# A fused attention, channel-mix and gated-convolution kernel: the second pair of chunks reordered, and half of a first-layer product placed inside the attention

## The chip, the cores and the metric

The kernel runs on 1 core of one Trainium2 chip (8 cores). The metric is the device time of one execution in microseconds (us); before the change it is 277.2 us, the median of 3 runs (276.21 to 277.38).

## The reference

Three layers follow one another on 2 sequences of 768 tokens, 512 features, in fp32.

```
# 1. linear attention with a decay per head; 8 heads of 64, blocks
intra = (q k^T * lam^(i-j), i>=j) v
inter = (q * lam^(i+1)) state
state = lam^block * state + (k * lam^(block-1-j))^T v
x     = intra + inter                      # (B, S, 512)
# 2. channel mix
xk = mu_k*x + (1-mu_k)*x_prev ; xr = mu_r*x + (1-mu_r)*x_prev
x2 = sigmoid(xr @ w_r) * (relu(xk @ w_k)**2 @ w_v)       # w_k: 512 x 1024
# 3. gated convolution
out = (sigmoid(conv5(x2)) * (x2 @ w_val)) @ w_out
```

## The kernel before

**Tiling.** The attention works on 12 chunks of 128 tokens (chunks 0 to 5 are the first sequence, 6 to 11 the second), two chunks being a pair p = 0 to 5. Everything behind it works on 3 tiles t of 512 tokens, so tile 0 needs pairs 0 and 1 alone. Each large product is done in three passes (`three_pass`, L714): every fp32 operand is split into a rounded high part and a low part (raw minus high), and high*high, low*high and high*low are added up in one PSUM bank. ScalarE (ACT) writes the high parts, VectorE (DVE) the low ones.

**Chunk n on TensorE (PE):** `scores(n)` (L725, 8 matmuls of k against q, two heads at a time), `update(n)` (L745, the new part of the state), `inter(n)` (L770, state times decayed q; none for chunks 0 and 6), `attend(n)` (L789, v times weighted scores). Chunks 5 and 11 have no update. Update n writes bank 6 (n even) or 7 (n odd). A pair's result lies in banks 4 and 5 (pair 5: 0 and 1) and is copied out by ACT (`evacuate_x`, L322).

**Chunk n on the other engines.** DVE: `weigh(n)` (L502, two 128x512 products that turn scores into pT) and `new_state(n)` (L512, faded state plus update). ACT: `fade(n)` (L333, four small activations that fade state n by the decay of a chunk). So the state goes update, new_state, fade, new_state, from chunk to chunk. GpSimd (POOL): `decay_k` and `decay_q` (L280, L291), which make kdec and qd from loaded k and q.

**Tile 0 of the channel mix** is prepared within the attention: `mix_part` (ACT, L346), `mix` (DVE, L527), `mix_high` (ACT, L358), `mix_low` (DVE, L535) make xk and its two parts for k = 0 to 3, and `high` (ACT, L341) and `low` (DVE, L540) split the weight piece by piece. Piece i of w_k serves output groups 2i and 2i+1 of `hidden(t, n)` (L810, 12 matmuls of 128x128 by 128x512; n = 0 to 7). `hidden(0, 0)` already stands between the halves of pair 5.

**What sets the order.** Each engine runs one stream written out by hand; engines meet at counting semaphores alone (`wait_ge`), and a waiting instruction holds all behind it on its engine. All loads are issued by SyncE on one queue in the order of the code (L229 to L262). DVE's stream in the attention is the loop at L630, ACT's is L418 to L447, PE's is L888 to L925. Behind the attention, PE runs hidden, `receptance` (L831) and `value` (L840) of the three tiles and then the last layer.

Of the kernel before, what the change touches and what calls it, by code (L numbers as in the profile page):

```python
# [9 lines left out]
ALU = mybir.AluOpType  # L10
# [25 lines left out]
TURNED = 7  # L36
OUT_FIRST = 4


# [13 lines left out]
def build(nc, prm_in, qk_in, v0_in, kv_in, w_k, w_v, w_r, w_val, w_out, out):  # L53
    with ExitStack() as ctx:
# [146 lines left out]
        def bank_of(kind, t, n):  # L201
            if kind == "mlp":
                return (2 * FT * t + n + 2) % 8
            place_of = [("val", 0), ("val", 1), ("proj", 0), ("val", 2), ("proj", 1), ("proj", 2)].index((kind, t))
            return (4 * place_of + n + 2) % 8
# [4 lines left out]
        def _(sp):  # L210
# [31 lines left out]
            for p in range(3, NP - 1):  # L242
                load_qk(2 * p)
                load_qk(2 * p + 1)
                load_kv(2 * p)
                load_kv(2 * p + 1)
            load_qk(NCH - 2)
            load_qk(NCH - 1)
            load_weight(wk_raw, w_k, 0, wk_here)
            load_kv(NCH - 2)  # L250
# [70 lines left out]
        def _(act):  # L321
            def evacuate_x(p):  # L322

                b, c = at(2 * p)
                cols = slice(b * SEG + HALO + c * CH, b * SEG + HALO + (c + 2) * CH)
                first = out_banks(2 * p)[0]
                act.wait_ge(att_done, 2 * p + 2)
                if p == OUT_FIRST:
                    act.wait_ge(inter_done, inters(2 * p + 1))
                nc.scalar.copy(x[:, :, cols].rearrange("p (g a) i -> p g a i", g=2),  # L330
                               ps[:, first:first + 2, :].rearrange("p g (a i) -> p g a i", a=2)).then_inc(x_ready, 1)
# [91 lines left out]
            fade(3)  # L423
            evacuate_x(1)
            fade(4)
            for k in range(KT):
                mix_part(0, k, 0)
            evacuate_x(2)
            fade(7)
            for k in range(3):  # L430
                mix_high(0, k, 0)
            fade(8)
            evacuate_x(3)
            high(wk, wk_raw, 0, wk_here, wk_hi)
            fade(9)
            mix_high(0, 3, 0)
            high(wk, wk_raw, 1, wk_here, wk_hi)
# [63 lines left out]
        def _(dve):  # L501
# [33 lines left out]
            def mix_low(t, k, which):  # L535
                to, raw, hi, lo = ((xk, xk_f, xk_hi, xk_lo), (xr, xr_f, xr_hi, xr_lo))[which]
                dve.wait_ge(hi, KT * t + k + 1)
                nc.vector.tensor_tensor(to[1][:, k, :], raw[:, k, :], f32(to[0][:, k, :]), ALU.subtract).then_inc(lo, 1)

            def low(w, raw, i, hi, lo):  # L540
                cols = slice(i * PIECE, (i + 1) * PIECE)
                dve.wait_ge(hi, i + 1)
                nc.vector.tensor_tensor(w[1][:, cols], raw[:, cols], f32(w[0][:, cols]), ALU.subtract).then_inc(lo, 1)
# [84 lines left out]
            dve.wait_ge(halo_ok, B)  # L628
            dve.wait_ge(om_ok, 1)
            for p in range(2, NP):  # L630
                new_state(2 * p)
                if p + 1 < NP:
                    weigh(2 * p + 2)
                    weigh(2 * p + 3)
                new_state(2 * p + 1)
                if p == 2:
                    mix(0, 0, 0)
                    mix(0, 1, 0)
                    mix(0, 2, 0)
                if p == 3:  # L640
                    mix(0, 3, 0)
                    mix_low(0, 0, 0)
                    mix_low(0, 1, 0)
                    mix_low(0, 2, 0)
                if p == 4:
                    mix_low(0, 3, 0)
                    low(wk, wk_raw, 0, wk_hi, wk_lo)
            for i in range(1, 4):
# [64 lines left out]
        def _(pe):  # L713
# [56 lines left out]
            def inter(n):  # L770
                b, c = at(n)
                if c == 0:
                    return
                pe.wait_ge(qd_ready, inters(n))
                pe.wait_ge(state_ready, updates(n - 1))
                if opens(n, True):
                    if n < NCH - 2:
                        pe.wait_ge(x_ready, n // 2)
                    else:
                        pe.wait_ge(p_ready, 2 * n + 2)  # L780
                for a in (0, 2, 1, 3):
                    for row in range(2):
                        last = nc.tensor.matmul(place_of(n, row, a), state[rows_of(row), n % 4, a * D:(a + 1) * D],  # L783
                                                qd[rows_of(row), n % 4, a * P:(a + 1) * P],
                                                start=(opens(n, True) and a % 2 == 0),
                                                stop=(n == 2 * OUT_FIRST + 1 and a % 2 == 1), skip_group_check=True)
                last.then_inc(inter_done, 1)

            def attend(n):  # L789
# [6 lines left out]
                for a in range(PAIRS):  # L796
                    for row in range(2):
# [3 lines left out]
                                                start=(opens(n, False) and a % 2 == 0),  # L801
                                                stop=(a % 2 == 1 and n % 2 == 1 and n // 2 != OUT_FIRST),
                                                skip_group_check=True)
                last.then_inc(att_done, 1)

            def wk_col(k, n):

                return n // 2 * PIECE + k * 2 * P + n % 2 * P

            def hidden(t, n):  # L810
                if n == 0:
# [3 lines left out]
                if t == 0 and n % 2 == 0:  # L815
                    pe.wait_ge(wk_lo, n // 2 + 1)
                if t == 0 and n == 2:
# [7 lines left out]
                elif t > 0:  # L825
                    pe.wait_ge(x2_ready, KT * (t - 1) + n - KT + 1)
                three_pass(ps[:, bank_of("mlp", t, n), :],
                           [(lambda z, k=k: wk[z][:, wk_col(k, n):wk_col(k, n) + P], lambda z, k=k: xk[z][:, k, :])
                            for k in range(KT)]).then_inc(h_done, 1)

            def receptance(t, m):  # L831
                if m == 0:
                    pe.wait_ge(xr_lo, KT * (t + 1))
                    pe.wait_ge(wr_lo, 2)
                pe.wait_ge(sq_ready, FT * t + m + 1)
                three_pass(ps[:, bank_of("mlp", t, FT + m), :],
# [64 lines left out]
            scores(4)  # L901
            update(2)
            scores(5)
            update(3)
            inter(3)
            attend(3)
            update(4)
            for p in range(2, NP):
                if p + 1 < NP:
                    scores(2 * p + 2)  # L910
                    scores(2 * p + 3)
                if p == OUT_FIRST:
                    attend(2 * p)
                    attend(2 * p + 1)
                inter(2 * p)
                if p + 1 == NP:
                    attend(2 * p)
                    hidden(0, 0)
                inter(2 * p + 1)
                if p not in (OUT_FIRST, NP - 1):  # L920
# [6 lines left out]
            for t in range(NT):  # L927
                for n in range(1 if t == 0 else 0, FT):
                    hidden(t, n)
                for m in range(KT):  # L930
                    receptance(t, m)
                for m in range(KT):
                    value(t, m)
# [66 lines left out]
```

## Time and profile before

| what | value |
|---|---|
| median of 3 runs | 277.2 us (276.21 to 277.38) |
| the profiled execution: its own time | 276.0 us |
| its span | 274.2 us |
| PE busy | 269.9 us, 98% |
| DVE, ACT, POOL busy | 166.0, 125.4, 23.6 us |
| granted TensorE clock | full in all 40 slices |
| mean DMA busy share in the 40 slices | 7 to 9 tenths in the first six, 6 in the seventh, then mostly 0 |

The span is the time from the first to the last instruction; the device time of the same execution is 1.8 us more. An engine's busy time counts the union of its instructions; matmuls overlap one another, so the distance from one start to the next tells what a matmul costs, not its length. In a timeline a row is a run of like instructions: its start, the time to its last end, and in brackets what ended the idle time before it.

### The profile page before, as it was taken

To read this page: it belongs to the slowest core of one execution; us is meant where nothing else is said; L and a number is where in the kernel's file an instruction comes from. 1 tells how busy PE (TensorE), PEld (TensorE's weight loads), DVE (VectorE), ACT (ScalarE), POOL (GpSimd) and SP (SyncE) were. 2 spreads that over 40 slices of the span, in tenths; PEclk is the share of its full clock that TensorE was granted. 3 is DMA by queue.
4 is the path that set the end of the run, shared out by engine and by line. 5 is a ranking of instruction groups with operands and counts; after the bars stand their busy time and mean duration, and the time that the engine had idled before them with its cause. 6 is when DMAs were issued, how large, how long until landed. Compare 5 with 4: busy or idle time off the path is not lost.

```text
span 274.2 us, 4270 instructions
## 1 busy us (share of the span) xinstructions
PE 269.9 (98%) x1746; PEld 226.3 (83%) x1746; DVE 166.0 (61%) x258; ACT 125.4 (46%) x223; POOL 23.6 (9%) x25
## 2 busy tenths in 40 slices
PE   8999999999999999999999999999999999999996
PEld 7889977888888888888888888888888888888886
DVE  5866999998581125465885553429969599325000
ACT  2237788977582124365721234748217306412121
POOL 1667750000000000000000000000000000000000
PEclk9999999999999999999999999999999999999999
DMA  7999996000000000000000000530000000310323
GB/s 215 408 410 406 406 407 253 0 0 2 0 0 0 2 0 0 0 2 0 0 0 2 2 0 0 174 134 0 0 0 2 0 0 0 117 38 0 115 82 111
DMA packets 7506, 22.57 MB, mean 82 GB/s; under 512 B 960, under 2 KB 1216, under 8 KB 7488
## 3 DMA queue, kind: packets, MB, share of 16 engines
q1 hardware_dynamic: 7488, 22.31, 21.4%
q8 instruction: 14, 0.23, 0.3%
q14 instruction: 4, 0.03, 0.0%
HBM read 19.16 MB, written 3.15 MB: 81 GB/s over the span
## 4 chain that ended last, share of the span: by engine, by line
PE 96%; DVE 2%; DMA 1%; issue 0%; ACT 0%
PE ps L717 28%; PE ps L719 28%; PE ps L718 28%; PE ps L799 4%; PE ps L733 4%; PE ps L783 2%; PE ps L761 2%; DMA prm<-in_prm 1%; DVE dec L608 1%; DVE pT L508 0%; DVE qdec L589 0%; ACT out_sb L414 0%
## 5 line engine op out<-in xcount | busy, mean ns | idle before, releaser
L717 PE MATMUL ps<-xk_h,wk_h 128*128 128x512 f32 x96 | 37.5, 391 | 0.0
L718 PE MATMUL ps<-xk_l,wk_h 128*128 128x512 f32 x96 | 37.4, 389 | 0.0
L719 PE MATMUL ps<-xk_h,wk_l 128*128 128x512 f32 x96 | 37.4, 389 | 0.0
L717 PE MATMUL ps<-kk_h,wv_h 128*128 128x512 f32 x96 | 37.3, 389 | 0.0
L718 PE MATMUL ps<-kk_l,wv_h 128*128 128x512 f32 x96 | 37.3, 389 | 0.0
L719 PE MATMUL ps<-kk_h,wv_l 128*128 128x512 f32 x96 | 37.3, 389 | 0.0
L571 DVE SCALAR_TENSOR_TENSOR gate<-x,prm,gate 128x512 f32<-128x512 f32 x48 | 32.6, 748 | 0.0
L547 DVE SCALAR_TENSOR_TENSOR kk_f<-ps,ring 128x512 f32<-128x512 f32 x24 | 16.6, 691 | 24.1 <-ACT ring L367 24.1
L384 ACT ACTIVATE gate<-x,prm 128x512 f32<-128x512 f32 x12 | 8.7, 725 | 43.2 <-DVE x L557 43.2
L367 ACT ACTIVATE ring<-ps 128x512 f32<-128x512 f32 x24 | 14.3, 597 | 26.7 <-PE ps L719 26.7
L717 PEld LDWEIGHTS ps<-xk_h,wk_h 128*128 128x128 f32 x96 | 18.0, 188 | 4.0 <-issue 0.3
L719 PEld LDWEIGHTS ps<-xk_h,wk_l 128*128 128x128 f32 x96 | 18.0, 188 | 3.8
L718 PEld LDWEIGHTS ps<-kk_l,wv_h 128*128 128x128 f32 x96 | 18.0, 188 | 3.8
L719 PEld LDWEIGHTS ps<-kk_h,wv_l 128*128 128x128 f32 x96 | 18.0, 188 | 3.8
L557 DVE TENSOR_TENSOR x<-ps,r 128x512 f32<-128x512 f32 x12 | 8.3, 690 | 21.1 <-PE ps L719 21.1
L718 PEld LDWEIGHTS ps<-xk_l,wk_h 128*128 128x128 f32 x96 | 18.0, 188 | 3.7
L717 PEld LDWEIGHTS ps<-kk_h,wv_h 128*128 128x128 f32 x96 | 18.0, 188 | 3.7
L719 PE MATMUL ps<-w_h,gl 128*128 128x512 f32 (+2 forms) x52 | 19.6, 376 | 0.0
L718 PE MATMUL ps<-w_l,gh 128*128 128x512 f32 (+2 forms) x52 | 19.6, 376 | 0.0
L717 PE MATMUL ps<-w_h,gh 128*128 128x512 f32 (+2 forms) x52 | 19.5, 375 | 0.0
L717 PE MATMUL ps<-xr_h,wr_h 128*128 128x512 f32 x48 | 18.7, 389 | 0.0
L718 PE MATMUL ps<-xr_l,wr_h 128*128 128x512 f32 x48 | 18.7, 389 | 0.0
(74 smaller groups left out, 487.5 us busy)
## 6 DMA issues: line engine op xcount, KB each, us to landing
qk<-in_qk SPq DMA_DIRECT2D x12, 512.0 KB, 11.3
kv<-in_kv SPq DMA_DIRECT2D x9, 512.0 KB, 12.8
out<-out_sb SPq DMA_DIRECT2D x11, 256.0 KB, 2.0
wk_raw<-in_w_k SPq DMA_DIRECT2D x4, 512.0 KB, 14.2
wv_raw<-in_w_v SPq DMA_DIRECT2D x4, 512.0 KB, 12.5
wr_raw<-in_w_r SPq DMA_DIRECT2D x2, 512.0 KB, 15.0
w_raw<-in_w_val SPq DMA_DIRECT2D x2, 512.0 KB, 4.4
w_raw<-in_w_out SPq DMA_DIRECT2D x2, 512.0 KB, 6.9
```

The source lines that it names most:

```text
L367: nc.scalar.activation(ring[:, n % 4, :], ps[:, bank_of("mlp", t, n), :], ACT.Relu).then_inc(relu_ready, 1)
L384: nc.scalar.activation(like(t, gate[t][:, k, :]), x_cols(t, k, HALO), ACT.Copy, scale=prm[:, col:col + 1]).then_inc(tap0, 1)
L547: nc.vector.scalar_tensor_tensor(out=kk_f[:, n, :], in0=ps[:, bank_of("mlp", t, n), :], scalar=0.0, in1=ring[:, n % 4, :], op0=ALU.max, op ...
L557: nc.vector.tensor_tensor(x_cols(t, m, 1), like(t, ps[:, bank_of("mlp", t, FT + KT + m), :]), like(t, r[:, m, :]), ALU.mult).then_inc(x2_r ...
L571: nc.vector.scalar_tensor_tensor(out=like(t, gate[t][:, k, :]), in0=x_cols(t, k, HALO - j), scalar=prm[:, col:col + 1], in1=like(t, gate[t ...
L717: nc.tensor.matmul(to, left(0), right(0), start=(i == 0), stop=False)
L718: nc.tensor.matmul(to, left(0), right(1), start=False, stop=False)
L719: done = nc.tensor.matmul(to, left(1), right(0), start=False, stop=(i == last))
L733: last = nc.tensor.matmul(ps_s[n % 2][row][:, cols], qk[i][rows_of(row), 1, cols], qk[i][rows_of(row), 0, cols], start=True, stop=True)
L761: last = nc.tensor.matmul(ps[rows_of(row), ps_u[n % 2], a * D:(a + 1) * D], kdec[:, n % 4, at_k:at_k + D], kv[i][:, 1, h * D:(h + 1) * D], ...
L783: last = nc.tensor.matmul(place_of(n, row, a), state[rows_of(row), n % 4, a * D:(a + 1) * D], qd[rows_of(row), n % 4, a * P:(a + 1) * P], ...
L799: last = nc.tensor.matmul(place_of(n, row, a), kv[i][:, 1, h * D:(h + 1) * D], pT[:, n % 4, row, a * P:(a + 1) * P], start=(opens(n, False ...
```

## The change

PE's order is changed for chunks 2 to 7: `attend(3)` and `inter(3)` (in this order) come before `scores(5)`, and `update(4)` goes between `scores(6)` and `scores(7)`. `inter(3)` now closes the second pair, so that its copy waits for `inter(3)` too (STATE_LAST). `hidden(0, 1)` is cut in two: the part over k = 0, 1 stands between `scores(11)` and `attend(8)`, that over k = 2, 3 behind `hidden(0, 0)`. Its bank becomes 7, the bank of update 9, so the first half waits for `new_state(9)`; group 5 takes bank 3 instead. The half also waits for two low parts of xk and for half of the first piece of w_k, which DVE now makes in two halves (`low_part`). On DVE, `mix` 0 and 1 come before `new_state(4)`, one `mix_low` before the products of 8, and `new_state(9)` before the products of 10. On ACT the copy of the second pair, the mixing and the casts move accordingly, and `fade(9)` moves ahead of the copy of pair 3. The first piece of w_k is loaded ahead of q and k of chunks 10 and 11.

```diff
@@ -35,6 +35,7 @@
...
 OUT_FIRST = 4
+STATE_LAST = (1, OUT_FIRST)
@@ -200,6 +201,8 @@
...
             if kind == "mlp":
+                if t == 0 and n in (1, 5):
+                    n = 6 - n
                 return (2 * FT * t + n + 2) % 8
@@ -244,9 +247,9 @@
...
                 load_kv(2 * p + 1)
+            load_weight(wk_raw, w_k, 0, wk_here)
             load_qk(NCH - 2)
             load_qk(NCH - 1)
-            load_weight(wk_raw, w_k, 0, wk_here)
             load_kv(NCH - 2)
@@ -325,7 +328,7 @@
...
                 act.wait_ge(att_done, 2 * p + 2)
-                if p == OUT_FIRST:
+                if p in STATE_LAST:
                     act.wait_ge(inter_done, inters(2 * p + 1))
@@ -422,18 +425,21 @@
...
             evacuate_x(1)
+            mix_part(0, 0, 0)
+            mix_part(0, 1, 0)
             fade(4)
-            for k in range(KT):
-                mix_part(0, k, 0)
+            mix_part(0, 2, 0)
+            mix_part(0, 3, 0)
             evacuate_x(2)
+            mix_high(0, 0, 0)
+            mix_high(0, 1, 0)
             fade(7)
-            for k in range(3):
-                mix_high(0, k, 0)
+            mix_high(0, 2, 0)
+            mix_high(0, 3, 0)
+            high(wk, wk_raw, 0, wk_here, wk_hi)
             fade(8)
+            fade(9)
             evacuate_x(3)
-            high(wk, wk_raw, 0, wk_here, wk_hi)
-            fade(9)
-            mix_high(0, 3, 0)
             high(wk, wk_raw, 1, wk_here, wk_hi)
@@ -537,6 +543,12 @@
...
+            def low_part(w, raw, i, half, hi, lo):
+
+                cols = slice(i * PIECE + half * PIECE // 2, i * PIECE + (half + 1) * PIECE // 2)
+                dve.wait_ge(hi, i + 1)
+                nc.vector.tensor_tensor(w[1][:, cols], raw[:, cols], f32(w[0][:, cols]), ALU.subtract).then_inc(lo, 1)
+
             def low(w, raw, i, hi, lo):
@@ -627,24 +639,29 @@
...
             dve.wait_ge(om_ok, 1)
+            mix(0, 0, 0)
+            mix(0, 1, 0)
             for p in range(2, NP):
                 new_state(2 * p)
+                if p == 3:
+                    mix_low(0, 0, 0)
+                if p == 4:
+                    new_state(2 * p + 1)
                 if p + 1 < NP:
...
                     weigh(2 * p + 3)
-                new_state(2 * p + 1)
+                if p != 4:
+                    new_state(2 * p + 1)
                 if p == 2:
-                    mix(0, 0, 0)
-                    mix(0, 1, 0)
                     mix(0, 2, 0)
+                    mix(0, 3, 0)
                 if p == 3:
-                    mix(0, 3, 0)
-                    mix_low(0, 0, 0)
                     mix_low(0, 1, 0)
+                    low_part(wk, wk_raw, 0, 0, wk_hi, wk_lo)
+                if p == 4:
                     mix_low(0, 2, 0)
-                if p == 4:
                     mix_low(0, 3, 0)
-                    low(wk, wk_raw, 0, wk_hi, wk_lo)
+                    low_part(wk, wk_raw, 0, 1, wk_hi, wk_lo)
             for i in range(1, 4):
@@ -783,7 +800,7 @@
...
                                                 start=(opens(n, True) and a % 2 == 0),
-                                                stop=(n == 2 * OUT_FIRST + 1 and a % 2 == 1), skip_group_check=True)
+                                                stop=(a % 2 == 1 and n % 2 == 1 and n // 2 in STATE_LAST), skip_group_check=True)
                 last.then_inc(inter_done, 1)
@@ -799,13 +816,38 @@
...
                                                 start=(opens(n, False) and a % 2 == 0),
-                                                stop=(a % 2 == 1 and n % 2 == 1 and n // 2 != OUT_FIRST),
+                                                stop=(a % 2 == 1 and n % 2 == 1 and n // 2 not in STATE_LAST),
                                                 skip_group_check=True)
...
                 return n // 2 * PIECE + k * 2 * P + n % 2 * P
+
+            def three_pass_of_part(to, pairs, opens, closes):
+                last = len(pairs) - 1
+                for i, (left, right) in enumerate(pairs):
+                    nc.tensor.matmul(to, left(0), right(0), start=(opens and i == 0), stop=False, skip_group_check=True)
+                    nc.tensor.matmul(to, left(0), right(1), start=False, stop=False, skip_group_check=True)
+                    done = nc.tensor.matmul(to, left(1), right(0), start=False, stop=(closes and i == last),
+                                            skip_group_check=True)
+                return done
+
+            def hidden_operands(t, n, ks):
+                return [(lambda z, k=k: wk[z][:, wk_col(k, n):wk_col(k, n) + P], lambda z, k=k: xk[z][:, k, :])
+                        for k in ks]
+
+            def second_hidden(half):
+
+                pe.wait_ge(xk_lo, (half + 1) * KT // 2)
+                pe.wait_ge(wk_lo, half + 1)
+                if half == 0:
+                    pe.wait_ge(state_ready, updates(NCH - 3))
+                done = three_pass_of_part(ps[:, bank_of("mlp", 0, 1), :],
+                                          hidden_operands(0, 1, range(half * KT // 2, (half + 1) * KT // 2)),
+                                          half == 0, half == 1)
+                if half == 1:
+                    done.then_inc(h_done, 1)
@@ -813,7 +855,7 @@
...
                 if t == 0 and n % 2 == 0:
-                    pe.wait_ge(wk_lo, n // 2 + 1)
+                    pe.wait_ge(wk_lo, n // 2 + 2)
                 if t == 0 and n == 2:
@@ -824,15 +866,13 @@
...
                     pe.wait_ge(x2_ready, KT * (t - 1) + n - KT + 1)
-                three_pass(ps[:, bank_of("mlp", t, n), :],
-                           [(lambda z, k=k: wk[z][:, wk_col(k, n):wk_col(k, n) + P], lambda z, k=k: xk[z][:, k, :])
-                            for k in range(KT)]).then_inc(h_done, 1)
+                three_pass(ps[:, bank_of("mlp", t, n), :], hidden_operands(t, n, range(KT))).then_inc(h_done, 1)
...
                     pe.wait_ge(wr_lo, 2)
-                pe.wait_ge(sq_ready, FT * t + m + 1)
+                pe.wait_ge(sq_ready, FT * t + m + 1 + (4 if (t, m) == (0, 1) else 0))
                 three_pass(ps[:, bank_of("mlp", t, FT + m), :],
@@ -900,15 +940,18 @@
...
             update(2)
+            attend(3)
+            inter(3)
             scores(5)
             update(3)
-            inter(3)
-            attend(3)
-            update(4)
             for p in range(2, NP):
...
                     scores(2 * p + 2)
+                    if p == 2:
+                        update(4)
                     scores(2 * p + 3)
+                if p == OUT_FIRST:
+                    second_hidden(0)
                 if p == OUT_FIRST:
@@ -916,6 +959,7 @@
...
                     hidden(0, 0)
+                    second_hidden(1)
                 inter(2 * p + 1)
@@ -925,7 +969,7 @@
...
             for t in range(NT):
-                for n in range(1 if t == 0 else 0, FT):
+                for n in range(2 if t == 0 else 0, FT):
                     hidden(t, n)
...
```

## Rows read from the trace of the kernel before

**Rows 1.** The page: busy time of each engine, then the instruction queue.
```profile
PE 269.9 (98%) x1746; PEld 226.3 (83%) x1746; DVE 166.0 (61%) x258; ACT 125.4 (46%) x223; POOL 23.6 (9%) x25
...
q8 instruction: 14, 0.23, 0.3%
```
**Rows 2.** Timeline of PE: start us, us, engine line op out<-in xcount [idle <-releaser].
```profile
14.86 1.09 PE L799 MATMUL ps<-pT,kv 128*64 128x128 f32 x16
15.88 1.16 PE L733 MATMUL ps<-qk 64*128 64x128 f32 x16
16.98 0.69 PE L761 MATMUL ps<-kv,kdec 128*64 128x64 f32 x16
17.59 1.16 PE L733 MATMUL ps<-qk 64*128 64x128 f32 x16
...
19.30 0.67 PE L783 MATMUL ps<-qd,state 64*64 64x128 f32 x16
19.89 1.09 PE L799 MATMUL ps<-pT,kv 128*64 128x128 f32 x16
...
23.37 1.10 PE L783 MATMUL ps<-qd,state 64*64 64x128 f32 x32
...
29.81 1.97 PE L799 MATMUL ps<-pT,kv 128*64 128x128 f32 x32
31.61 1.10 PE L761 MATMUL ps<-kv,kdec 128*64 128x64 f32 x32
...
34.63 0.66 PE L799 MATMUL ps<-pT,kv 128*64 128x128 f32 x8
35.89 1.53 PE L799 MATMUL ps<-pT,kv 128*64 128x128 f32 x24 [0.61 <-issue]
37.35 1.10 PE L783 MATMUL ps<-qd,state 64*64 64x128 f32 x32
```
**Rows 3.** Timeline of PE: hidden(0, 0), then inter(11), and the first receptance.
```profile
40.65 0.47 PE L717 MATMUL ps<-xk_h,wk_h 128*128 128x512 f32 x1
...
43.24 0.39 PE L719 MATMUL ps<-xk_h,wk_l 128*128 128x512 f32 x1
43.55 0.67 PE L783 MATMUL ps<-qd,state 64*64 64x128 f32 x16
...
64.35 0.39 PE L717 MATMUL ps<-xr_h,wr_h 128*128 128x512 f32 x1
```
**Rows 4.** Timeline of DVE, same columns.
```profile
18.30 0.41 DVE L525 TENSOR_TENSOR state<-faded,ps 128x256 f32<-128x256 f32 x1
...
28.91 2.47 DVE L508 TENSOR_TENSOR pT<-ps,dec 128x512 f32<-128x512 f32 x4
...
31.62 0.91 DVE L532 SCALAR_TENSOR_TENSOR xk_f<-x,om,xk_f 128x512 f32<-128x512 f32 x1
32.46 2.96 DVE L538 TENSOR_TENSOR xk_l<-xk_f,xk_h 128x512 fp32r<-128x512 f32 x3
...
46.97 2.74 DVE L532 SCALAR_TENSOR_TENSOR xr_f<-x,om,xr_f 128x512 f32<-128x512 f32 x4 [0.45 <-ACT xr_f L355]
...
60.29 0.69 DVE L538 TENSOR_TENSOR xr_l<-xr_f,xr_h 128x512 fp32r<-128x512 f32 x1
```
**Rows 5.** Timeline of ACT, same columns.
```profile
26.42 1.02 ACT L330 COPY x<-ps 128x1024 f32<-128x1024 f32 x1 [0.95 <-PE ps L799]
29.02 1.07 ACT L338 ACTIVATE faded<-state,qdec 128x64 f32<-128x64 f32 x4 [1.58 <-DVE state L522]
29.99 1.65 ACT L361 CAST xk_h<-xk_f 128x512 fp32r<-128x512 f32 x3
...
33.60 1.05 ACT L344 CAST wk_h<-wk_raw 128x1024 fp32r<-128x1024 f32 x1
```
**Rows 6.** Timeline of POOL, same columns.
```profile
28.42 2.32 POOL L286 TENSOR_TENSOR kdec<-kv,dec 128x512 f32<-128x512 f32 x2 [1.65 <-DMA kv<-in_kv]
30.70 2.97 POOL L298 TENSOR_TENSOR qd<-qk,qdec 128x512 f32<-128x512 f32 x2
```

## The prediction

> **What bounds the kernel now.** I read the busy times first: PE is busy 98% of the span, DVE 61% [rows 1]. So the end moves only if PE's stream gains or loses idle time or work. Next PE's own timeline, looking for places where the distance from one start to the next exceeds its usual value. In the attention there is one large place. The output products of 8 and 9 take from 34.63 to 37.35, 2.72 us; those of 6 and 7, the same 32 matmuls, take 29.81 to 31.61, 1.80 us [rows 2]. About 0.10 of the excess is the dearer switch to an inter product (an attend before scores costs 15.88 - 14.86 = 1.02, a lone one before an update some 0.92). The rest, **0.82 us**, is the hole after the eighth matmul, which the profile puts on "issue": no semaphore released it. The queue that fetches instructions moves 14 packets of 16 KB (0.23 MB) in the span [rows 1]; a packet every 256 instructions of a stream with 1746 matmuls and 1746 weight loads is PE's own program. I take the hole for a late packet, fetched while the loads keep DMA full. Behind the attention PE waits for nobody, so what is won or lost before 43.55 is passed on to the end.
>
> **The sum, part by part.** It is made on the profiled execution (276.0 us), in PE starts.
>
> *The reordered chunks 2 to 7.* Before, scores(4) to inter(4) is 23.37 - 15.88 = 7.49 [rows 2]. Unit prices from starts: scores 1.09 (15.88 to 16.98), update 0.61 (16.98 to 17.59), inter 0.60 (19.30 to 19.89), attend 1.02. The new order holds three more lone pieces and fewer twins: scores 4, update 2, attend 3, inter 3, scores 5, update 3, scores 6, update 4, scores 7 = 4*1.09 + 3*0.61 + 1.02 + 0.60 = 7.81. That is **+0.33** for switching. No row shows inter followed by scores or update by attend; the nearest switches cost 0 to 0.15 more than a run without one, so each of these two is open by 0.1 either way.
>
> *A new wait at inter(3).* It needs the state made from update 2, which DVE writes from 18.30 to 18.71 [rows 4]; its gates are all older than the change. PE now reaches inter(3) at 15.88 + 1.09 + 0.61 + 1.02 = 18.61, and a first matmul comes 0.14 after its state (in the same trace 10.94 to 11.08). So it starts at 18.85: **+0.24**. Bounds 0 and 0.3. PE is now 0.57 late.
>
> *Inter(5)* is next at 24.45. DVE has two mixes (0.67 apart [rows 4]) ahead of new_state(4): products of 5 until 21.9, new_state(3), the small scale, mixes from 22.3, new_state(4) done at 24.1. This holds, by 0.2, if the second mix begins before POOL takes its kdec of 6. Cost 0; the other bound is 0.8.
>
> *The first half of hidden(0, 1)* is where the change is decided. PE could begin it at 34.63 + 0.57 = **35.20**. It waits for new_state(9), and that is the end of a chain on DVE and ACT:
> - The copy of pair 2 follows attend(5), so it moves from 26.42 to 27.0 [rows 5]; the first cast of xk (0.6 long) ends at 28.54. Kdec of 8 starts at 28.42 as before, since it waits for its load [rows 6].
> - DVE against POOL: three low parts from 32.46 took 2.96 us [rows 4], where three at 0.60 apart would take 1.88. POOL's two qd run until 33.67 in 2.97 [rows 6] instead of 2*1.27. So each side sat until the other's instruction ended, then came the other's turn; a blocked low part or mix ends 0.55 after POOL's (31.62 + 0.91 = 32.53, POOL's qd ended at 31.98). The products with a PSUM operand (2.47 for four, 0.60 apart) ran unhindered beside POOL.
> - So mix_low(0, 0), ready at 28.57, sits until kdec of 8 ends at 29.48: done 30.03. Then four products at 0.60 and new_state(7): 29.95 + 2.40 = 32.35, done 32.76 (before: 31.70).
> - POOL, pushed by this, runs kdec of 9 to 30.96, qd of 8 to 32.2, qd of 9 to 33.4. Thus mix_low(0, 1), issued at 32.7, is blocked until then and ends at 34.0; low_part (same size) ends 34.6; new_state(8) 34.5 to 34.9. Had mix_low(0, 0) slipped in ahead of kdec of 8, low_part would be the one blocked, and new_state(8) would start at 34.7: the place is firm.
> - fade(9) takes 1.07 [rows 5]: 34.93 to 36.0. new_state(9), which waits for it, starts 0.12 later and takes 0.41: 36.5. First matmul 36.68.
>
> The wait is 36.68 - 35.20 = **+1.48**. Bounds: 0 if POOL and DVE never met (the same chain then ends near 35.05), 2.2 if the first cast of w_k is no earlier than before (33.60, done 34.65 [rows 5]), which delays low_part by some 0.7. I take 1.48: load and cast have two 512 KB loads less ahead of them and I expect the cast at 31.0. What is queued behind the waiting half on PE: attend(8) and all the rest, so nothing hides it.
>
> The six matmuls cost what they cost in the dense stretch ((43.24 - 40.65)/11 = 0.235 with its start [rows 3]), so they are moved and not added: 0. A switch out of them is added: 43.55 - 43.24 = 0.31 against 0.23: **+0.08**.
>
> *The hole of 0.82.* Its packet is due a fixed count of instructions into the stream, so it now falls some four instructions into attend(8), at about 38.2, while the fetch was asked for only 0.57 later than before. It arrives during DVE's wait: **-0.82**. Were it still late: 0.
>
> *Loads, ACT and the rest.* Scores(10) moves to 33.2, so its loads, one piece later each, have time. The copy of pair 3 now stands behind fade(9), done at 37.0; attend(8) comes at 38.2. For hidden(0, 0), at 43.4, DVE's last low parts are there by 40.7. Inter(11) moves from 43.55 by 0.57 + 1.48 + 0.08 - 0.82 + 2*1.4 = 4.1, and with it the copy of pair 5, the mixing of xr and the squares. Its last low part moves from 60.29 + 0.69 = 60.98 to at most 65.1; receptance, at 64.35, moves to 65.65 [rows 3, 4]. Margin 0.5, no wait. Receptance 1, which now wants the sixth square because of the exchanged bank, has 1.5.
>
> **Sum:** 0.33 + 0.24 + 1.48 + 0.08 - 0.82 = **+1.3 us**. On the profiled 276.0 that is 277.3; the median of the runs shown stands 1.2 above that execution, so I forecast 277.2 + 1.3 = **278.5 us**. About 0.5% (1.4 us) is what a measurement of this kernel can tell from no change.
>
> **The page's view.** The Trainium skill, page "SBUF — State Buffer", section "Who interferes with whom", says that a VectorE instruction with two SBUF inputs and a GpSimd one that reads SBUF exclude each other for a whole instruction, and that the one issued first holds the ports. By that rule the two blocked low parts come as in my chain; the trace agrees, with the 2.96 us for three low parts [rows 4]. The page "Runtime: NRT & Kernel Launch", section "Instruction fetch mechanics", says that fetching in blocks of 256 instructions is mostly hidden. By that rule the hole would be something else and could stay in the new order; the trace has a hole of 0.82 with no other releaser.
>
> **Rivals.**
> 1. *The state chain is in time.* For it: DVE gets through its low parts before POOL's qd, with loads that land a little otherwise. Against: POOL's 2.97 us [rows 6] cover just the stretch where these low parts now stand. The sum loses 1.48: -0.2, so 277.0.
> 2. *Not slower but faster by more than it can be told apart.* The hole is longer in executions without much luck in the fetches (the runs differ by 1.2 us), and the cover takes it away in all: rival 1 with a hole of 2 instead of 0.8, -1.4, so 275.8. It decides if PE begins the half before about 35.3 and the median hole exceeds 2. Against: the chain, and the profiled hole.
> 3. *More on the chain.* The second mix loses its place to kdec of 6, or the cast of w_k comes at 33.6: new_state(9) is 0.4 to 0.7 later: +1.7 to +2.0, so 279.0. It decides from about 0.1 us beyond my sum.
> 4. *The hole is no late fetch, or is late again.* It then stays: +2.1, so 279.3. For it: nothing shows what the packet waited for.
>
> **How the numbers follow.** Forecast 0.52, rival 1 0.18, rival 2 0.05, rival 3 0.17, rival 4 0.08. The forecast's own spread of 0.6 lies on both sides of the 1.4 us bound: 0.32 of its 0.52 below it and 0.20 above. Rival 1 is within the bound but for 0.02 that its median shows faster. So faster 0.07, within 0.5% 0.48, slower 0.45. The range 276.9 to 279.6 takes in rivals 1, 3 and 4 and leaves out rival 2 and the tails.
>
> **What would show it.** In the changed profile: inter(3) behind a short wait of about 0.2 for the state; scores(11) followed by a wait of PE of 1 to 2 us, ended by DVE's state at about 36.5; on DVE two low parts longer than 1 us between 28.5 and 34; no hole within attend(8); receptance starting near 65.6. The forecast is wrong if the six matmuls start before 36.0, if DVE passes POOL without being held, or if PE waits somewhere behind 45.

## The result, and the profile after

| | before | changed |
|---|---|---|
| median of 22 runs each | 276.99 us (275.87 to 277.85) | 277.41 us (277.20 to 278.30) |
| ratio of the runs | | 1.0032, 95% interval 1.0022 to 1.0043 |
| the profiled execution | 276.0 | 277.29 |
| its last matmul starts at | 271.63 | 272.93 |

The changed kernel is slower by 0.3%, in a forecast that gave 278.5 us in 276.9 to 279.6. Between the two profiled executions the difference is 1.29 us, close to the prediction's sum of 1.3; between the medians it is 0.42 us, and between the lowest times 1.33 us. The experiments are on why these three differ. One execution of the changed kernel in a later run, 281.81 us, was in a slower state and is left out of the ratios, which compare fast executions alone.

First, PE's timeline in the changed kernel, with the columns of [rows 2]:

```profile
16.91 0.68 PE L778 MATMUL ps<-kv,kdec 128*64 128x64 f32 x16
17.43 1.04 PE L816 MATMUL ps<-pT,kv 128*64 128x128 f32 x16
18.79 0.67 PE L800 MATMUL ps<-qd,state 64*64 64x128 f32 x16 [0.32 <-DVE state L531]
...
23.89 1.10 PE L800 MATMUL ps<-qd,state 64*64 64x128 f32 x32
...
32.14 1.30 PE L778 MATMUL ps<-kv,kdec 128*64 128x64 f32 x32
33.36 2.06 PE L750 MATMUL ps<-qk 64*128 64x128 f32 x32
36.56 0.47 PE L830 MATMUL ps<-xk_h,wk_h 128*128 128x512 f32 x1 [1.14 <-DVE state L531]
...
38.10 1.97 PE L816 MATMUL ps<-pT,kv 128*64 128x128 f32 x32
40.00 1.10 PE L800 MATMUL ps<-qd,state 64*64 64x128 f32 x32
...
65.65 0.39 PE L734 MATMUL ps<-xr_h,wr_h 128*128 128x512 f32 x1
```

See the half product at 36.56, forecast 36.68, after a wait for DVE's state: 36.56 less its unhindered start, 33.36 + 1.99 = 35.35, is 1.21 us. Attend(8) and (9) now run through, 38.10 to 40.00 = 1.90 us, where they took 2.72 [rows 2]. Receptance starts at 65.65, as the sum said (64.35 before [rows 3]).

The chain that the wait is for, first on DVE, then on POOL (before: [rows 4, 6]):

```profile
28.51 1.37 DVE L544 TENSOR_TENSOR xk_l<-xk_f,xk_h 128x512 fp32r<-128x512 f32 x1
29.80 2.47 DVE L514 TENSOR_TENSOR pT<-ps,dec 128x512 f32<-128x512 f32 x4
32.20 0.41 DVE L531 TENSOR_TENSOR state<-faded,ps 128x256 f32<-128x256 f32 x1
32.52 1.31 DVE L544 TENSOR_TENSOR xk_l<-xk_f,xk_h 128x512 fp32r<-128x512 f32 x1
33.75 0.68 DVE L550 TENSOR_TENSOR wk_l<-wk_raw,wk_h 128x512 fp32r<-128x512 f32 x1
34.36 0.41 DVE L531 TENSOR_TENSOR state<-faded,ps 128x256 f32<-128x256 f32 x1
35.99 0.42 DVE L531 TENSOR_TENSOR state<-faded,ps 128x256 f32<-128x256 f32 x1 [1.23 <-ACT faded L341]
```

```profile
28.27 1.06 POOL L289 TENSOR_TENSOR kdec<-kv,dec 128x512 f32<-128x512 f32 x1 [1.30 <-DMA kv<-in_kv]
29.55 1.25 POOL L289 TENSOR_TENSOR kdec<-kv,dec 128x512 f32<-128x512 f32 x1 [0.21 <-DMA kv<-in_kv]
30.77 2.51 POOL L301 TENSOR_TENSOR qd<-qk,qdec 128x512 f32<-128x512 f32 x2
```

The two low parts of xk (xk_l) take 1.37 and 1.31 us, and each ends 0.55 after an instruction of POOL (POOL's end at 29.33 and 33.28), while the half low part of w_k, of the same size, takes 0.68. The last line waits 1.23 us for ACT's fade.

### The profile page after: what moved, and what is told of

The parts are those of the page before. It is cut to its first block, busy times and chain, and to the rows that moved or that the text cites. A ratio compares the mean times of both kernels' runs of the same rounds, so it can differ in the third digit from the quotient of the medians.

```text
span 275.5 us, 4274 instructions
## 1 busy us (share of the span) xinstructions
PE 271.0 (98%) x1746; PEld 227.0 (82%) x1746; DVE 165.3 (60%) x259; ACT 125.6 (46%) x223; POOL 23.2 (8%) x25
## 4 chain that ended last, share of the span: by engine, by line
PE 86%; DVE 4%; issue 1%; ACT 0%; DVEq 0%
PE ps L734 28%; PE ps L735 27%; PE ps L736 27%; DVE pT L514 2%; PE ps L816 1%; DVE xk_f L538 1%; PE ps L800 1%; DVE state L531 1%; DVE xk_l L544 0%; PE ps L830 0%; ACT faded L341 0%; PE ps L831 0%; PE ps L832 0%; DVE wk_l L550 0%; PE ps L778 0%
## 5 line engine op out<-in xcount | busy, mean ns | idle before, releaser
L734 PE MATMUL ps<-xk_h,wk_h 128*128 128x512 f32 x92 | 36.0, 392 | 0.0
L736 PE MATMUL ps<-xk_h,wk_l 128*128 128x512 f32 x92 | 35.8, 389 | 0.0
L735 PE MATMUL ps<-xk_l,wk_h 128*128 128x512 f32 x92 | 35.8, 389 | 0.0
L734 PEld LDWEIGHTS ps<-xk_h,wk_h 128*128 128x128 f32 x92 | 17.3, 188 | 3.9 <-issue 0.3
L736 PEld LDWEIGHTS ps<-xk_h,wk_l 128*128 128x128 f32 x92 | 17.3, 188 | 3.6
L735 PEld LDWEIGHTS ps<-xk_l,wk_h 128*128 128x128 f32 x92 | 17.3, 188 | 3.5
L735 PE MATMUL ps<-x2l,w_h 128*128 128x512 f32 x48 | 18.7, 389 | 0.0
```

Source lines behind the costliest of these rows:

```text
L734: nc.tensor.matmul(to, left(0), right(0), start=(i == 0), stop=False)
L735: nc.tensor.matmul(to, left(0), right(1), start=False, stop=False)
L736: done = nc.tensor.matmul(to, left(1), right(0), start=False, stop=(i == last))
```

## The experiments

A "hole" is a long distance between two matmul starts with no releaser, and its size is that whole distance; an unhindered one is 0.05 to 0.1. "At the 961st instruction" means that the hole follows the 961st, counting PE's weight loads, matmuls and separate waits in the order of their records. A "packet" is one 16 KB transfer of the instruction queue. Two medians are compared within one job where the text says "beside"; a comparison with the changed kernel's 277.41 goes across jobs.

**The kernel before, twice more.** No edit.

> The kernel before, unchanged, profiled once more. Theory: its executions differ by how late PE's instruction packet is in attend(8); the first profile (276.0 us) was a short one, and one near the median (277.0) shows the same PE starts up to 34.6 and a hole of about 1.8 us instead of 0.82 there. Rival: the slower executions lose their 1 us elsewhere (at the start, waiting for the first loads, or in the last layer), and the hole is 0.8 in all of them.

> The kernel before, unchanged, once more, so that a short and a long execution are likely to be among the profiles. Theory: time minus hole is the same in all profiles of it (276.0 - 0.8 = 275.2) within 0.2 us. Rival: the time varies with the hole unchanged.

Measured: 275.79 and 277.39 us. PE's timeline of the short one, then of the long one:

```profile
32.38 2.06 PE L733 MATMUL ps<-qk 64*128 64x128 f32 x32
34.37 0.66 PE L799 MATMUL ps<-pT,kv 128*64 128x128 f32 x8
35.59 1.53 PE L799 MATMUL ps<-pT,kv 128*64 128x128 f32 x24 [0.57 <-issue]
```

```profile
27.23 1.83 PE L733 MATMUL ps<-qk 64*128 64x128 f32 x28
30.10 0.49 PE L733 MATMUL ps<-qk 64*128 64x128 f32 x4 [1.04 <-issue]
...
35.93 0.66 PE L799 MATMUL ps<-pT,kv 128*64 128x128 f32 x8
37.27 0.98 PE L799 MATMUL ps<-pT,kv 128*64 128x128 f32 x14 [0.68 <-issue]
```

The last line ends with the window that was asked for, and so counts 14 of the 24 matmuls. The hole in attend(8) is 0.84 and 0.95 (0.88 in the first profile): it hardly varies, so my theory (this hole grows) fell. The long execution has a second one, 1.31 us, inside scores(9). Both lie at fixed places of the stream, the 961st and the 1217th instruction, 256 apart. Time less the holes is 275.0 and 275.1, and 275.1 in the first profile, so the second theory stands in the form: time = about 275.1 + holes. The packet ahead of the long execution's hole at 961 is alone in its window of 27.3 to 28 us, where the data queue keeps DMA full:

```profile
q1 hardware_dynamic: 77, 0.27, 98.1%
q8 instruction: 1, 0.02, 9.6%
```

**The changed kernel, again, and once more with more runs.** No edit.

> The changed kernel, unchanged, profiled once more. Theory: PE waits for DVE's state of 9 before the half product in every execution (matmul at 36.4 to 36.8, wait 1.2 us) and has no hole in attend(8), so the time is 277.2 to 277.5. Rival: the wait itself varies by 1 us from one execution to another.

> The changed kernel, unchanged, beside new executions of the kernel before. Theory (the sum of 1.3 us holds between executions without a hole at the 961st instruction, and such a hole costs the changed kernel little since its wait covers it): lowest against lowest 1.2 to 1.4 us; medians differ by 0.4 to 1.3, by how often the kernel before has that hole this time; the changed kernel's own lower half lies within 0.3 us. Rival (the two kernels differ by 0.4 us in all executions): lowest against lowest 0.3 to 0.6.

Measured: 277.65 us for the first; for the second a median of 277.49 (277.24 to 278.39, and the 281.81 named above) beside 276.79 (275.63 to 277.88), ratio 1.0031, interval 1.0013 to 1.0049; lowest against lowest +1.61, past my 1.4. PE of the first:

```profile
24.55 1.10 PE L800 MATMUL ps<-qd,state 64*64 64x128 f32 x32 [0.63 <-issue]
...
28.41 1.83 PE L750 MATMUL ps<-qk 64*128 64x128 f32 x28
31.00 0.49 PE L750 MATMUL ps<-qk 64*128 64x128 f32 x4 [0.76 <-issue]
...
34.85 2.06 PE L750 MATMUL ps<-qk 64*128 64x128 f32 x32
36.84 0.50 PE L830 MATMUL ps<-xk_h,wk_h 128*128 128x512 f32 x1
```

Here PE has holes of 0.90 at the 705th (the expectation of the state chain below calls it the 706th) and 1.04 at the 961st instruction and then finds the state ready: 34.85 + 1.99 = 36.84, no wait. So my theory of a wait in every execution fell, and the rival held: the wait itself varies. The two holes cost 0.36 us in time against the execution without them, because the wait and the holes cover each other.

The second run was profiled in an execution of 278.06 us. It too has holes (0.81 at the 705th, 1.04 at the 961st) and a half product that starts within 0.1 of its unhindered start, yet it is 0.77 longer than the execution without holes. It was 0.34 behind already at inter(3) (19.13 against 18.79), where POOL's qd came last and not the state:

```profile
19.13 0.67 PE L800 MATMUL ps<-qd,state 64*64 64x128 f32 x16 [0.48 <-POOL qd L301]
```

POOL makes this qd right after its kdec of 3, which waited for its load until 16.78 (15.89 in the first profile of the changed kernel).

**The instruction stream shifted.** The kernel before with

```diff
-            for _ in range(WARM):
-                nc.tensor.matmul(ps[:, 7, 0:P], ones, ones, start=True, stop=True)
+            for _ in range(2 * WARM):
+                nc.tensor.matmul(ps[:, 7, 0:P // 2], ones, ones[:, 0:P // 2], start=True, stop=True)
```

> The kernel before with 18 warm-up matmuls of 64 columns instead of 9 of 128: 36 more instructions ahead of the first scores, the same work. If the hole is a late block of 256 instructions, it moves 36 instructions forward in the stream, from after the eighth matmul of attend(8) to inside scores(11), about 0.6 us earlier in PE's work (start near 34.0), and it stays or grows by up to 0.5 us, since the stream gets there sooner. Rival (attend(8) waits for something of its own, a load or a semaphore): the hole stays after the eighth matmul of attend(8). Time within 0.5 us of before.

Measured: 282.42 us, where I had expected a time within 0.5 us of before. The 64-column matmuls start 0.21 us apart like those of 128 columns did, so that the first scores start at 8.62 instead of 4.88, 3.7 of the 5.9 us; the scores and turning products up to 14.25 took 1.1 longer as well, for a reason that I did not trace, and the holes are larger (0.73 and 1.54). On the disputed point it is clear:

```profile
32.05 0.93 PE L733 MATMUL ps<-qk 64*128 64x128 f32 x11
33.44 1.49 PE L733 MATMUL ps<-qk 64*128 64x128 f32 x21 [0.46 <-issue]
...
38.41 1.60 PE L733 MATMUL ps<-qk 64*128 64x128 f32 x23
41.28 0.82 PE L733 MATMUL ps<-qk 64*128 64x128 f32 x9 [1.27 <-issue]
```

The hole has left attend(8) and lies within scores(11), still at the 1217th instruction; the other is still at the 961st. It belongs to the count, not to the work. And in every profile with such a hole PE goes on 2.35 to 2.62 us after the start of an instruction packet. That settles that the packet is late, though not why.

**POOL's part cut.** The changed kernel, with part of qd of 8 and 9 and of kdec of 8 left out:

```diff
+                    wide = 1 if n == 8 else H
...
+                    wide = P // 8 if n in (8, 9) else DM
                     nc.gpsimd.tensor_tensor(
-                        qd[:, n % 4, :], qk[i][:, 0, :],
...
+                        qd[:, n % 4, 0:wide], qk[i][:, 0, 0:wide],
```

The first `wide` counts the heads of kdec, the second the columns of qd (P is 128, DM 512).

> The changed kernel with POOL's qd of chunks 8 and 9 cut to 16 of 512 columns and kdec of 8 to one head of 8 (the rest of these tiles is left out). Theory (two of DVE's low parts are held by POOL, 0.7 us each): both take 0.7 us instead of 1.3 to 1.4, new_state(8) starts 1.2 to 1.4 us earlier unless fade(8) holds it, the half product starts at about 35.4 instead of 36.56, PE's wait before it shrinks from 1.2 to under 0.2 us, and an execution without other holes is 1.0 to 1.2 us shorter (276.1 to 276.3). Rival (the chain is set by the fades and the order on ACT alone): low parts shorter, but the half product still starts after 36.2 and the time is the same within 0.3.

Measured: 277.04 us (275.97 to 278.33). DVE:

```profile
28.26 0.80 DVE L546 TENSOR_TENSOR xk_l<-xk_f,xk_h 128x512 fp32r<-128x512 f32 x1
...
32.16 0.69 DVE L546 TENSOR_TENSOR xk_l<-xk_f,xk_h 128x512 fp32r<-128x512 f32 x1
...
33.60 0.42 DVE L533 TENSOR_TENSOR state<-faded,ps 128x256 f32<-128x256 f32 x1
```

Both low parts are short and the state of 8 comes 0.76 earlier (DVE also waited 0.37 for scores that a hole delayed). PE has no wait before the half, but that is not the cut alone. The profile has a hole of 1.04 at the 961st instruction; without it PE would have been there 0.98 earlier (34.95 instead of 35.93), and the state, which ended at 35.67, 0.37 earlier at most. So I estimate that 0.5 to 0.9 of the 1.21 would be left, where under 0.2 was forecast. The lowest time is 1.23 below the changed kernel's, about as forecast, but the median 0.37 only, which neither theory said.

**The half product moved back**, beside its other half; the copy of pair 3 ahead of fade(9):

```diff
                 if p == OUT_FIRST:
-                    second_hidden(0)
-                if p == OUT_FIRST:
                     attend(2 * p)
...
                     hidden(0, 0)
+                    second_hidden(0)
                     second_hidden(1)
```

> The changed kernel with the first half of hidden(0, 1) moved back beside the second, behind hidden(0, 0), and the copy of pair 3 back ahead of fade(9) on ACT; the reordering of chunks 2 to 7 stays. Theory: PE no longer waits before the half (-1.2) but meets the hole at the 1217th instruction again, in attend(8), some 0.5 us (its packet comes as before and PE is 0.6 later): 276.5 to 276.8, that is 0.6 to 0.9 less than the changed kernel and 0.5 more than the profile of before. Rival (the half product in that place is what fills the hole and pays): slower than the changed kernel by 0.3 or more.

Measured: 277.63 us (276.55 to 278.58), where 276.5 to 276.8 was forecast. The hole at 1217 is back, 0.61 (some 0.5 forecast), and the lowest time is 0.65 below the changed kernel's. But the median is not better. The profiled execution took 277.2; its inter(3) waited 0.9 us for POOL's qd, 0.6 more than in the first profile of the changed kernel, and nothing covers the hole. That this holds for the other executions is not shown. So the place of the half is neither what costs (at the median) nor what pays.

**PE's order of chunks 2 to 7 as before**, with the second pair's copy waiting for attend alone, the rest as changed:

```diff
-            attend(3)
-            inter(3)
             scores(5)
             update(3)
+            inter(3)
+            attend(3)
+            update(4)
...
-                    if p == 2:
-                        update(4)
```

> The changed kernel with PE's order of chunks 2 to 7 as before (inter(3) and attend(3) after update(3), update(4) before scores(6), the second pair's copy waiting for attend alone); DVE, ACT, POOL and the half product stay as changed. Theory (the reordering costs 0.6 us on PE but feeds ACT's copy of the second pair 1.3 us sooner, which DVE's new place for the first two mixes needs): the copy comes at about 21.0 instead of 19.65, the first mix at 22.7, the second is held by POOL's kdec of 6, new_state(4) ends at about 25.3, inter(5) waits for it 1.4 us, the half product starts at 37.4 to 37.8, and the time is 0.8 to 1.2 us more than the changed kernel's. Rival (the reordering is a pure cost): 0.5 to 0.6 less than the changed kernel.

Measured: 278.11 us (277.67 to 279.23), beside 276.08; that is 0.7 more than the changed kernel's median, where 0.8 to 1.2 was forecast. DVE, then PE:

```profile
23.03 2.22 DVE L538 SCALAR_TENSOR_TENSOR xk_f<-x,om,xk_f 128x512 f32<-128x512 f32 x2 [1.96 <-ACT xk_f L358]
25.17 0.41 DVE L531 TENSOR_TENSOR state<-faded,ps 128x256 f32<-128x256 f32 x1
```

```profile
23.45 0.67 PE L800 MATMUL ps<-qd,state 64*64 64x128 f32 x16
25.73 0.67 PE L800 MATMUL ps<-qd,state 64*64 64x128 f32 x16 [1.60 <-DVE state L531]
```

Each step of the expectation is there, some 0.3 later than forecast: mixes late, the pair at 2.22 instead of 1.41 beside POOL's kdec, the state at 25.6, inter(5) waiting 1.6. The profiled execution (278.63) also has holes, of 1.03 at the 449th and 1.31 at the 961st instruction. The reordering on PE is a cost that the new order on DVE makes necessary.

**The state chain brought forward.** The changed kernel with new_state(7) between the products of 8 and 9, new_state(8) ahead of the half low part, and on POOL:

```diff
...
+            decay_k(8)
+            decay_k(9)
+            decay_k(10)
+            for n in range(8, NCH):
+                decay_q(n)
```

> The changed kernel with the state chain brought forward: on DVE new_state(7) between the products of 8 and 9 and new_state(8) ahead of the half low part of w_k; on POOL kdec of 10 and then all qd of 8 to 11, so that no qd runs while DVE makes low parts. Theory: new_state(8) done by 33.6, fade(9) by 34.6, new_state(9) by 35.1, so the half product starts at 35.4 without a wait, and its 1.4 us cover the hole in attend(8): 1.2 us less than the changed kernel, 276.1 to 276.4, and a median 0.5 to 0.8 below that of before. Rival (holes elsewhere, at the 706th and 961st instruction, are then no longer covered by the wait): the lowest times fall by 1.2 but the median by 0.3 to 0.6 alone.

Measured: 277.13 us (276.36 to 279.08); ratio to before 1.0018 (0.9997 to 1.0039), where a median 0.5 to 0.8 below before's was forecast. The second low part takes 0.67 (the first, still beside kdec, 1.60), and nothing waits before the half product, though new_state(8) came at 34.0, held 0.74 by an update that a hole had delayed. The lowest time is 0.84 below the changed kernel's, the median 0.28: nearest to the rival. The hole in its profile:

```profile
27.59 1.83 PE L761 MATMUL ps<-qk 64*128 64x128 f32 x28
30.50 0.49 PE L761 MATMUL ps<-qk 64*128 64x128 f32 x4 [1.08 <-issue]
```

**Loads held back**, in the kernel before (twice) and in the last version:

```diff
+            sp.wait_ge(att_done, IN_BUFS)
+            sp.wait_ge(update_done, updates(IN_BUFS - 1))
             for i in range(1, 4):
                 load_weight(wk_raw, w_k, i, wk_here)
+            sp.wait_ge(att_done, IN_BUFS + 2)
             for i in range(2):
                 load_weight(wr_raw, w_r, i, wr_here)
-            sp.wait_ge(att_done, IN_BUFS)
-            sp.wait_ge(update_done, updates(IN_BUFS - 1))
```

> The kernel before with the loads of pieces 1 to 3 of w_k issued only once attend(7) and update(7) are done (about 31.8 instead of 22.8) and those of w_r after attend(9). The loads' queue stays filled, but there are 6 us less of it ahead of a new packet when PE asks for the block that starts at its 1217th instruction. Theory (the packet is late because of the depth of the loads' queue): the packet goes out before 31.5 instead of 33.4, the hole of 0.8 goes, time -0.8. Rival (the packet's delay doesn't depend on how many loads are queued, only on DMA being busy): packet at 33.4 and the hole as before, time the same within 0.3.

> The kernel before with the held loads, again, with more executions, to tell 0.4 us from nothing. Theory (hole at the 1217th instruction 0.7 smaller, the one at the 961st as often as before): median 0.3 to 0.6 below before, highest below 277.1, lowest no lower than before's. Rival: nothing gained, ratio 1.000 within 0.001.

> The version with the state chain brought forward (v_all), and the loads of pieces 1 to 3 of w_k and of w_r held back as in e_held. Theory: what is left in v_all against before is 0.3 for switching, 0.4 to 0.6 at inter(3), and a hole at the 961st instruction in some executions, which the held loads can't reach (they start later): median within 0.3 of v_all (277.1), lowest 276.3. Rival (the depth of the queue sets all fetches behind 20 us): median below 276.5.

Measured: 276.49 us beside 276.92, ratio 0.9991 (0.9974 to 1.0007); again 276.05 beside 276.08, ratio 0.9993 (0.9976 to 1.0010); in the last version 276.94 beside 276.08, ratio 1.0018 (0.9998 to 1.0038). In the kernel before, the forecast gains of 0.8 and of 0.3 to 0.6 did not come; the second time it is the rival, nothing gained.

The packet for the block that starts at 1217 starts 3.6 to 4.0 us after PE enters the block ahead of it, instead of 4.6 to 4.75, and the hole there is 0.13 or none in the two profiles of the kernel before:

```profile
35.33 2.05 PE L800 MATMUL ps<-pT,kv 128*64 128x128 f32 x32
```

But both of these have the hole at 961 (1.04, 1.31), so that their packets still start at 33.5 and 33.2 and not before 31.5. An execution with neither hole would take about 275.1; the lowest of the 22 is 275.79. What was won at 1217 was thus lost elsewhere, in the two profiles at 961, and why is open. The last version was profiled in an execution without any hole (276.3); there PE waits 0.20 for the state before the half product and 0.40 for the low part of w_k, whose load is now held:

```profile
35.13 0.47 PE L842 MATMUL ps<-xk_h,wk_h 128*128 128x512 f32 x1 [0.20 <-DVE state L539]
```

A gain is not shown, and no version tried is shown to be faster than the kernel before.

## Why the prediction was right, and where it was not

- *The sum* held on the profiled execution: +1.3 forecast, +1.29 measured. That it fits so closely is luck in part. The half product started 0.12 earlier than forecast (36.56 against 36.68), from errors of +0.15 and -0.27 that are told below, and the switches behind it made up the difference.
- *Reordered chunks with inter(3)'s wait*: 0.33 (7.81 - 7.49 is 0.32) + 0.24 forecast; measured 0.59, inter(4) 23.89 against 23.37 and the changed kernel 0.07 ahead when it came to this part. Update followed by attend costs 0.52, not 0.61, and the wait at inter(3) takes that up. The prediction gave this wait one gate, the state. It has a second, POOL's qd of 3, which in the kernel before ended at 18.46, 0.25 ahead of the state; in five of the seven profiles of the new order that gate came last, with 0.3 to 0.9 us of idle time.
- *Wait before the half product*: 1.48 forecast, 1.21 measured. Kdec of 8 came 0.15 earlier in this execution, and PE stood at 35.35 instead of 35.20: updates 8 and 9 took 1.22 us from start to start instead of 1.03, since update(9) waited for new_state(7), whose bank it takes, a wait that I had not listed. That POOL holds DVE's two low parts is shown by the cut; that it is the whole of the wait is not.
- *Hole of 0.82 gone*: yes, as forecast, and that a late packet makes it is settled. Why the packet is late is not. Of the Trainium skill's "Runtime: NRT & Kernel Launch", section "Instruction fetch mechanics", the blocks of 256 instructions are borne out. That fetching is mostly hidden holds by count (14 packets in the span, at most two holes in any profile), but in this attention the exceptions cost the kernel before 0.8 to 1.3 us each.
- *Inter(5), hidden(0, 0), receptance without a wait*: yes.
- *The step that failed* is the last one, "the median of the runs shown stands 1.2 above that execution, so I forecast 277.2 + 1.3". I took the distance from profile to median for a constant that the change leaves alone. What the profiles show in its place is a hole at the 961st instruction that some executions of the kernel before have and the profiled one had not: time less holes is nearly constant. The changed kernel waits for DVE behind that place, so that the same hole costs it little: 277.65 with it (and one at the 705th), 277.29 without, where the kernel before has 277.39 and 275.79. Hence 1.3 between executions without that hole, and 0.4 to 0.7 between medians. That this hole sets the medians is argued from three profiles of each kernel and from the times: of the 22 of the kernel before, seven lie at 275.87 to 276.30 and the others at 276.69 or more, with none between (in later jobs the gap is less clean). How often the hole occurs is not shown.
- *Rival 2* had the right idea with the wrong sign: the variation of the holes matters, but it was the wait, not the half product, that took it up. *Rival 4* is out.

## What to carry to other kernels

Before adding a sum to a median, ask what the profiled execution lacked that the median has, and whether the changed kernel would feel it: a wait and a stall close ahead of it cost about the larger of the two, not both (here 1.94 us of holes in place of a wait of 1.21 cost 0.36 more). Where a step is put in to fill a stall, follow the chain of its own inputs first; here it needed a state 1.2 us later than the stall offered its place. Count every reordering of small products: the switches added here (0.33 us forecast) come to 40% of the stall that was to be filled.

## What the runs showed of the hardware

- While the loads keep DMA full (406 to 410 GB/s from 7 to 41 us in the kernel before), a packet of PE's instructions starts 2.3 to 2.9 us after PE enters the block before, or 3.5 to 6.2 us; for one and the same block (at 961) both occur, from execution to execution. In each profile with a hole PE goes on 2.35 to 2.62 us after the packet's start. A block of 256 instructions of small matmuls (5.6 us from the 705th to the 961st) hides the first and not the second.
- Matmuls of a 128x64 fp32 operand followed one another at 0.21 us, just like those of 128x128, in the warm-up.
- A low part on DVE that meets POOL ends 0.55 us after POOL's instruction, and POOL's next one takes longer in turn: kdec of 9 took 1.25 us instead of 1.06.
